# Loading the first keys straight into the Gram blocks' buffers, moving the first key products behind them, and moving the gate work behind block 8

## What is computed

```python
# 1. delta-rule attention, B=4, H=8, S=768, D=48
k_n = k / (np.linalg.norm(k, axis=-1, keepdims=True) + 1e-06)
state = np.zeros((B, H, D, D))
for t in range(S):
    kt, vt, bt = k_n[:, :, t], v[:, :, t], beta[:, :, t, None]
    y[:, :, t] = np.einsum('bhd,bhde->bhe', q[:, :, t], state)
    v_old = np.einsum('bhde,bhd->bhe', state, kt)
    state = state + bt[:, :, :, None] * np.einsum('bhd,bhe->bhde', kt, vt - v_old)
# 2. x = y as (3072, 384); h = x @ w_in (2048 wide); g = ELU(h); x = g @ w_out
# 3. top-2 of 8 experts on noisy logits; out += weight * relu(x @ w1[e]) @ w2[e]
```

## Time and profile before

| | |
|---|---|
| median of 3 runs | 1170.54 us (1169.98 to 1171.93) |
| the profiled execution's own time | 1170.35 us |
| its span, first to last instruction | 1168.6 us |
| busy share of the span: TensorE matmul, VectorE, ScalarE, GpSimd | 96%, 55%, 40%, 30% |
| start of the attention's main loop (first `solve`) | 79.59 us |
| mean DMA traffic over the span | 117 GB/s |

### The profile page before, as it was taken

How to read it: one execution, slowest core, us unless ns; L and a number is a source line. 1 busy time by engine, 2 the same in 40 slices (tenths; PEclk the granted TensorE clock), 3 DMA queues, 4 the chain that set the end, 5 groups by cost and what they waited for, 6 DMA issues and landing times.

```text
span 1168.6 us, 29044 instructions
## 1 busy us (share of the span) xinstructions
PE 1116.6 (96%) x11562; PEld 1069.0 (91%) x11562; DVE 647.9 (55%) x1552; ACT 462.5 (40%) x1048; POOL 355.3 (30%) x378
## 2 busy tenths in 40 slices
PE   4898999899999999999999999999999999999996
PEld 3886787778999999999999999999999999999995
DVE  4989788663455646465565647533534343434342
ACT  1236665784333333433333345423333333333331
POOL 4289995542002021020202012322222232322223
PEclk9999999999999999999999999999999999999998
DMA  7553556855997011110101011472424242424221
GB/s 158 127 126 93 132 120 155 220 159 199 370 358 241 21 48 41 35 41 20 41 20 41 15 50 65 172 231 76 165 74 173 76 168 84 157 97 145 62 70 53
DMA packets 82603, 137.30 MB, mean 117 GB/s; under 512 B 11050, under 2 KB 70034, under 8 KB 81466
## 3 DMA queue, kind: packets, MB, share of 16 engines
q1 hardware_dynamic: 68490, 87.97, 25.9%
q0 software_dynamic: 12992, 28.75, 7.6%
q10 hardware_dynamic: 1008, 18.97, 4.3%
HBM read 81.96 MB, written 53.77 MB: 116 GB/s over the span
## 4 chain that ended last, share of the span: by engine, by line
PE 74%; DVE 1%; issue 0%; ACT 0%; POOL 0%; ACTq 0%; POOLq 0%
PE ps_x L1409 18%; PE ps_x L1499 18%; PE ps_h L1398 17%; PE ps_h L1477 17%; PE ps_r L1457 2%; PE ps_r L1448 2%; DVE hg L1817 0%; ACT hg L1607 0%; POOL out_dram L1364 0%; DVE w_parts L1780 0%; PE ps_r L1516 0%; DVE x_raw L1810 0%; PE ps_r L1426 0%; ACT yT_d L1625 0%; PE ps_r L1424 0%
## 5 line engine op out<-in xcount | busy, mean ns | idle before, releaser
L1499 PE MATMUL ps_x<-hg,w_parts 128*128 128x400 f32 x1152 | 230.2, 346 | 0.0
L1409 PE MATMUL ps_x<-w_parts,hg 128*128 128x400 f32 x1152 | 229.7, 346 | 0.0
L1398 PE MATMUL ps_h<-xg,w_parts 128*128 128x384 f32 x1152 | 222.3, 338 | 0.0
L1477 PE MATMUL ps_h<-xg,w_parts 128*128 128x400 f32 x1116 | 220.6, 345 | 1.1 <-DVE w_parts L1780 1.1
L1409 PEld LDWEIGHTS ps_x<-w_parts,hg 128*128 128x128 f32 x1152 | 209.6, 188 | 0.0
L1817 DVE SCALAR_TENSOR_TENSOR hg<-ps_h,hg 128x400 fp32r<-128x400 f32 x128 | 73.6, 575 | 243.1 <-ACT hg L1607 242.6
L1398 PEld LDWEIGHTS ps_h<-xg,w_parts 128*128 128x128 f32 x1152 | 204.0, 188 | 2.5 <-DVE elu_parts L1674 2.5
L1477 PEld LDWEIGHTS ps_h<-xg,w_parts 128*128 128x128 f32 x1116 | 202.7, 188 | 4.0 <-issue 3.1
L1499 PEld LDWEIGHTS ps_x<-hg,w_parts 128*128 128x128 f32 x1152 | 206.0, 188 | 0.0
L1344 POOL DMA_INDIRECT xs_scratch<-x,rows_now x48 | 49.2, 1025 | 393.5 <-DVE rows_now L1754 293.9
L1607 ACT ACTIVATE hg<-ps_h 128x400 fp32r<-128x400 f32 x128 | 64.6, 505 | 256.4 <-PE ps_h L1477 256.4
(11 more groups left out here) (175 smaller groups left out, 1312.4 us busy)
## 6 DMA issues: line engine op xcount, KB each, us to landing
xs_scratch<-pads SPq DMA_DIRECT2D x2, 5502.0 KB, 42.4
x_rows<-xs_scratch SPq DMA_DIRECT2D x17, 614.1 KB
kqT<-in_kqT_dram SPq DMA_DIRECT2D x48, 192.0 KB, 4.0
carried<-in_w_dram ACTq DMA_DIRECT2D x3, 3072.0 KB, 10.9
w_raw<-in_w_dram ACTq DMA_DIRECT2D x3, 3072.0 KB, 11.3
xs_scratch<-pads SPq DMA_DIRECT2D x6, 1375.5 KB, 17.0
out_dram<-pads SPq DMA_DIRECT2D x1, 4800.0 KB, 30.3
xs_scratch<-pads SPq DMA_DIRECT2D x6, 786.0 KB, 8.9
```

The costliest lines, as they stand in the source:

```text
L1398: mm = nc.tensor.matmul(ps_h[f % 2][:, 0:TB], wi[:, a, k, f * P:(f + 1) * P], xr[:, b, k, :], start=(i == 0), stop=(i == len(passes) - 1))
L1409: mm = nc.tensor.matmul(ps_x[t][:, 0:DG], act_r[:, f % RING, a, t * P:(t + 1) * P], wo[:, b, f, :], start=(f == 0 and i == 0), stop=(f == ...
L1477: mm = nc.tensor.matmul(ps_h[f % 2][:, 0:TR], w1, xg[:, b, k, :], start=(m == 0), stop=(m == len(passes) - 1))
L1499: mm = nc.tensor.matmul(ps_y[k][:, 0:TR], w2r[i][:, a, s, k * P:(k + 1) * P], hg[:, s % RING, b, :], start=(s == 0 and m == 0), stop=(s == ...
```

## The change

- Loads: kT(0) and kT(1) go first, then the beta moves, kT(2), kT(3), kqT(0), beta, kqT(1); kT(4) and on wait on `chunk_done` as before.
- TensorE: block 0 reads its keys from kT(0). The first four key products go behind blocks 3, 4, 5 and 6.
- ScalarE copies these four products from PSUM (`take_products`, two copies each), and GpSimd multiplies them by the masks in place, where VectorE did both in one. The first root (`root_of(0)`) goes behind `take_blocks(3)`, the second behind the copy of gate step 1.
- Gate work: four steps behind each of the blocks 8 to 11, in place of two behind each from block 5 on.
- VectorE breaks off after 8 columns of group 0 (`PREPARED`), not 12.
- One of the two `keep_clock(256)` goes.

```diff
-PREPARED = 12
+PREPARED = 8
 KEEP_BUSY = 29
+GATE_FROM = 8
+W_CHUNKS = 4
...
+        def kept_keys(n, c, h):
+            return lq[n % KEPT].rearrange("p (g a h) s t -> p g a h (s t)", g=2, h=2)[:, :, c * QP // 2:(c + 1) * QP // 2, h]
+
+        def mask_of_keys():
+            return masks[:].rearrange("p g s t -> p g (s t)").unsqueeze(2).to_broadcast([P, 2, QP // 2, 2 * P])
...
         def chunks_with(i):
-            at = 2 * (i - KT_BUFS - 1)
-            return (at, at + 1) if at >= 0 else ()
+            at = W_CHUNKS * (i - GATE_FROM)
+            return range(at, min(at + W_CHUNKS, FT1)) if at >= 0 else ()
...
+            load_kT(0)
             load_kT(1)
-            for n in range(2):
-                sp.wait_ge(kqT_cleared, n + 1)
-                load_kqT(n)
...
             load_kT(2)
-            for i in range(3, KT_BUFS + 1):
-                sp.wait_ge(chunk_done, i - 2)
-                load_kT(i)
+            load_kT(3)
+            sp.wait_ge(kqT_cleared, 1)
+            load_kqT(0)
             sp.wait_ge(beta_moved, 48)
             sp.dma_start(beta_sb[:].rearrange("p s i -> p (s i)"), beta_turned).then_inc(beta_loaded, 16)
-            for i in range(KT_BUFS + 1, NIT // 2):
+            sp.wait_ge(kqT_cleared, 2)
+            load_kqT(1)
+            for i in range(KT_BUFS, NIT // 2):
...
+            pool.wait_ge(masks_cleared, 1 + 2 * (NR - 1 + 2))
+            for n in range(2):
+                for c in range(2):
+                    for h in range(2):
+                        pool.wait_ge(grams_taken, (2 * n + c) * 2 + h + 1)
+                        nc.gpsimd.tensor_tensor(kept_keys(n, c, h), kept_keys(n, c, h), mask_of_keys(), ALU.mult
+                                                ).then_inc(masked, 1)
             pool.wait_ge(cleared, len(by_pool))
             for n in range(2):
                 scale_v(n)
...
             for i in range(NIT // 2):
-                if i < 4:
-                    products_of_keys(i // 2, i % 2)
                 diagonal_blocks(i)
+                if 0 <= i - 3 < 4:
+                    products_of_keys((i - 3) // 2, (i - 3) % 2)
                 gate_work(i)
-            gate_work(NIT // 2)
...
             pe.wait_ge(from_lanes, 1)
             keep_clock(256)
-            keep_clock(256)
...
+            def take_products(n, c):
+                act.wait_ge(grams_done, 2 * n + c + 1)
+                for h in range(2):
+                    nc.scalar.activation(kept_keys(n, c, h), of_keys(h).rearrange("p g a s t -> p g a (s t)"), ACT.Copy
+                                         ).then_inc(grams_taken, 1)
...
             for i in range(NIT // 2):
-                if i == 4:
+                take_blocks(i)
+                if i == 3:
                     root_of(0)
-                if i == 8:
-                    root_of(1)
-                take_blocks(i)
+                if 0 <= i - 3 < 4:
+                    take_products((i - 3) // 2, (i - 3) % 2)
                 for f in chunks_with(i):
                     take_turned(f)
-            for f in chunks_with(NIT // 2):
-                take_turned(f)
+                    if f == 1:
+                        root_of(1)
...
             nc.vector.memset(lane_t[0], 0.0).then_inc(zeros_set, 1)
-            dve.wait_ge(masks_cleared, 1 + 2 * (NR - 1 + 2))
-            mask_products(0, 0)
-            mask_products(0, 1)
-            mask_products(1, 0)
-            mask_products(1, 1)
             to_set_lanes(0, (0, 1))
```

More of the change, by code:

```diff
@@ L172, in attention_outputs @@
         grams_done = sem("grams_done_a")
+        grams_taken = sem("grams_taken")
         masked = sem("masked")
@@ L444, in diagonal_blocks @@
             def diagonal_blocks(i):
[L446 to L450, removed]
+                pe.wait_ge(kT_loaded[i % KT_BUFS], i // KT_BUFS * 32 + 32)
+                if i:
                     pe.wait_ge(blocks_taken, i)
@@ L457, in diagonal_blocks @@
                         for h in range(2):
[L458 to L461, removed]
+                            k_u = kT[heads(h), i % KT_BUFS, ca // QP, a, rows_of(r)]
                             mm = nc.tensor.matmul(ps_d[rows_of(to), h, ca * BLK:(ca + 1) * BLK], k_u, k_u,
@@ L490, in gate_work @@
                         pe.wait_ge(wgn_loaded, 16)
-                        pe.wait_ge(masked, 8)
+                        pe.wait_ge(grams_taken, 8)
                     turn_output_weights(f)
@@ L501, in products_of_keys @@
                     pe.wait_ge(products_cleared, 1)
+                elif n < 2:
+                    pe.wait_ge(grams_taken, (2 * n + c) * 2)
                 else:
@@ L909, in mask_products @@
                 for h in range(2):
-                    to = lq[n % KEPT].rearrange("p (g a h) s t -> p g a h (s t)", g=2, h=2)[:, :, c * QP // 2:(c + 1) * QP // 2, h]
-                    nc.vector.tensor_tensor(to, of_keys(h).rearrange("p g a s t -> p g a (s t)"),
-                                            masks[:].rearrange("p g s t -> p g (s t)").unsqueeze(2).to_broadcast([P, 2, QP // 2, 2 * P]),
+                    nc.vector.tensor_tensor(kept_keys(n, c, h), of_keys(h).rearrange("p g a s t -> p g a (s t)"), mask_of_keys(),
                                             ALU.mult).then_inc(masked, 1)
```

1 line of the change is left out of this document (removed).

## The result

The changed kernel takes 1181.97 us (median of 4 runs, 1180.66 to 1184.02) against 1171.24 for the kernel before in the same runs: a ratio of 1.0103 on record, 95% interval 1.008 to 1.0125 (the two medians alone give 1.0092). By the medians it is slower by 10.7 us, where 4.6 had been forecast and 1180 was the upper end of the range. The profiled execution took 1180.66, 10.3 more than the one of before.

A forecast was written before the change was run, and what follows sets the result against it. TensorE, busy 96% of the span, was taken as the bound: gate work 5.1 later less 0.94 starts the loop 4.2 later; with v's shift 4.6 was taken, giving 1175.1 us, range 1173 to 1180 (0.60), wider range 1166 to 1180.

The forecast's parts named there:

- Blocks 0 to 3: TensorE's first blocks: block 0 starts at 5.1 us, block 3 ends at 22.0 and is copied by 22.7.
- F: Price of refilling TensorE's instruction stream, restart to restart: taken as 3.6 to 5.7 us, more with DMA traffic.
- VectorE: Its chain before the main loop: gains 2.7 us at block 3, reaches column 8 at 37.4.
- Worth nothing: The eight masked copies taken off VectorE: no gain; on GpSimd hidden, at most 8 x 1.2 = 10 us.
- Gate work: Sixteen steps behind block 8's end at 45.2: 35.1 us, ending at 80.3, 5.1 later than before.
- One `keep_clock(256)` less: The matmuls ahead of the first solve: 3.06 us in place of 4.0, so 0.94 comes back.
- Sum: Main loop starts at 83.8 us, 4.2 later; v(2) and v(3) 5.1 later; 4.6 taken in all.
- 1: Rival: refills stay quick at 3.6 us each although loads come forward; -4.5, 1166 us; chance 0.15.
- 2: Rival: break-even, mean refill near 4.1 us; shift -0.7 to +0.2, 1170 us; chance 0.13.
- 3: Rival: refills are hidden, blocks go at the pace of landings and copies; loop 7 earlier, 1163 us; chance 0.05.
- 4: Rival: upper clock comes late after the shorter dense stretch; up to 4 us per pair, 1179 us; chance 0.07.
- 5: Rival: worst traffic, refills of 5.85 six times and 3.6 twice; loop +8.8, 1179 to 1180, the forecast's upper end.

The follow-up runs named there:

- lean run: The changed kernel with kT(0) to kT(3) loaded at once, then no loads until three blocks are done: 1179.98 us, ratio 1.0068.
- backlog run: The kernel before with four weight tiles (0.8 MB) loaded right behind kT(2) in place of later: 1172.91 us, ratio 1.0018.
- v late: The kernel before with v(2) and v(3) issued only when solve(0, 1) is done: 1174.02 us, ratio 1.0027.
- v early: v(2) and v(3) loaded ahead of the wait for the last turned tile: in the changed kernel 1177.64 us, in the kernel before 1169.28 us.
- after_metered: The changed kernel with the first loads given out in steps, kT(3) waiting for one block, later loads for more: 1176.93 us, ratio 1.0063.
- after_gate7: The changed kernel with the gate work one block earlier (GATE_FROM = 7), behind blocks 7 to 10: 1179.87 us, ratio 1.0075.

## Why the prediction was wrong

The mechanism at the start and the sign were right, the size was less than half of the measured one, and the path by which the loop hangs on the start was not the one assumed. Step by step:

- *Blocks 0 to 3.* Start at 5.0 (forecast 5.1) and the places of the stalls: right. The step that failed is F: "I take F = 5.3, 5.5 and 4.5 (bounds 3.5 and 5.9)". Measured 4.8, 9.6 and 6.3. I took F as a price per traffic share, and the longest refill in the rows of before, with the share at its full 1.12, as its bound. The lean run and the backlog run show that what counts is what stands in the queues when the piece is asked for, and what is issued right behind. Over the eight refills the sum was 41.0, not 37.7, the start of the first 0.2 earlier, so block 8 ended 3.1 late (48.3, forecast 45.2).
- *VectorE.* Block 3 was copied at 28.0 and not 22.7, so this chain lost 2.7 where I had it gain 2.7. It was covered: the second root ran at 51.1 behind the first two gate steps, and the first half of `place` (81.84 and 3.68 for both) was done at 83.7, just ahead of the gate work's end at 84.2, as forecast. "Worth nothing" for the masks was right for the end, but GpSimd took 10.7 us for the eight, over the bound of 10, and they were not free: see the last section.
- *Gate work.* From block 8's end to its own 35.9, forecast 35.1. Right but for a block 9 of 1.86 and a stall of 0.36.
- *One `keep_clock(256)` less.* 3.14 instead of 4.00 us on TensorE, 0.86 of the 0.94 forecast, but worth nothing in the time.
- *Sum.* The second step that failed: "The main loop starts ... 4.2 later" was taken as the term, and v only as a small correction "up to 5.1. I take 4.6". The loop of both kernels is paced by GpSimd's elimination, which stands still until v(3) is there. From the scaling of v(3) to the ELU stage it took 194.2 us before, 193.6 after, and 192 to 195 in the seven further kernels with the old place of v that ran before the one with v late (196.4 in that one, at a mean granted clock of 0.992 over the span, the lowest of all); from the first `solve` it took 198 to 204 in the same nine. The v of the changed kernel came 10.65 later: 9.0 by the gate work's end, in front of which its loads can't be issued, and 1.65 that their issue and landing took longer. That second part varies by itself: v(3) was scaled 10.5 to 12.6 us behind the gate work's end in the eight kernels with the same turns and loads in front of v (10.85 before, 12.51 in the changed kernel, 11.1 in it with the `keep_clock` put back). So of the 5.7 missed in the profiled execution 3.9 are the gate work's end (3.1 refills, 0.8 steps), 1.65 the way of v, and 0.5 that I took 4.6 and not the 5.1 of v; the rest of the kernel gave 0.3 back.
- *Rivals.* 1, 2 and 3 are out: the mean of the eight refills was 5.1. 4 is out: the products behind the first `solve` took 0.88. The level is read from that length alone, also in the prediction's "the trace agrees": the granted clock is 1.00 both from 8 to 10 us, where 16 products take 1.56, and from 88 to 90 in the changed kernel, where they take 0.88. 5 had the right place, the refills, but its bound of 5.85 for each was the wrong kind of bound: one refill alone took 9.6.

What stays open: why loads that are issued half a microsecond behind a request still move ahead of its packet, so that a refill takes 6.0 to 6.6 with an empty queue at its request. Also open is what order of loads, if any, would keep all refills at 3.5: the ones tried only moved the traffic.

## What to carry to other kernels

Where an engine has hundreds of tiny instructions in a row, look for "issue" stalls at even counts of instructions: its instruction stream is then a load like any other, queued with the data, and loads brought forward can hold up the engine that they were to feed. Before costing a shift of a stage's start, find which wait paces the stage: here it was a load issued behind the old work, and moving that load alone made the kernel before 2.0 us faster, while a first `solve` 2.2 us later (`PREPARED` = 8) cost it nothing that can be measured.

## What the runs showed of the hardware

- The page counts the instruction packets of queue 8, the queue in which TensorE's refills were found: in both kernels 83 packets of 16 KB.

```profile
q8 instruction: 83, 1.36, 0.5%
```

- A refill of TensorE's stream of 256 instructions took 3.4 to 3.7 us in quiet queues, 6.0 to 6.6 with an empty queue at the request and loads issued right behind it, and 9.0 to 11.0 with some 0.9 MB of loads outstanding at the request, in the four kernels that had that (9.6 in the changed kernel, 11.0 in it with v early); in other traffic up to 7.0. In quiet queues the 3.5 us are 1.1 until the packet starts, 1.0 for the packet and 1.4 until TensorE goes on (in the changed kernel five DMAs of 192 KB were issued from 6.82 to 10.4 us and landed 6.2 to 6.3 behind their issue, so that none of them was there at the request at 10.84).
- Small operations of VectorE grew up to five times while GpSimd masked products in SBUF beside them: the four 128x64 multiplications of group 0's norms, 0.22 and 0.23 us in the kernel before, took 1.29, 1.19, 0.66 and 1.20 here. Group 1's four, from 52.04 on, with GpSimd idle, took 0.22 and 0.23 in the same trace. The reciprocal at 33.98, which stands between them and also ran beside GpSimd, took 0.55 as in the kernel before. Timelines of DVE and of POOL in the changed kernel:

```profile
31.20 1.29 DVE L869 TENSOR_TENSOR inversion<-inversion 128x64 f32<-128x64 f32 x1
```

```profile
31.14 2.49 POOL L429 TENSOR_TENSOR carried<-carried,masks 128x512 f32<-128x512 f32 x2 [15.86 <-ACT carried L738]
```

It shows in the traces of the changed kernel's variants too (1.29 and 1.19 again in `after_metered`, `after_lean`, `after_gate7`), but no run here took GpSimd away from the same operations.
